# The first layer of a fused feed-forward, over pairs of token tiles with seven block products in place of eight

## The chip, the cores and the metric

The kernel runs on one core of a Trainium2 chip. The metric is the device time of one execution in microseconds (us); lower is better. TensorE (PE in the rows, PEld for its weight loads) does the matrix products, VectorE (DVE), ScalarE (ACT) and GpSimd (POOL) do elementwise work, and SyncE (SP) issues all DMAs.

## The reference

```python
# attention with decay: B, H, S, D = 4, 8, 768, 64
state = gamma * state + k_t (outer) v_t ;  y_t = scale * q_t @ state
x = y in the layout [3072 tokens, 512]
# first feed-forward, w_in [512, 1024], w_out [1024, 512]
h = x @ w_in
sm = softmax(h) ; solu = h * sm
ln = (solu - mean) / sqrt(var + 1e-6) * g_ln
y = ln @ w_out
# second feed-forward, w_in [512, 2048], w_out [2048, 512]
out = ((y @ w_in2) * cos(y @ w_in2)) @ w_out2
```

## The kernel before

There are two stages. Stage one takes the 3072 tokens in 24 tiles of 128 (4 sequences of 6 tiles) through attention and the first feed-forward, and stores y, transposed, to a scratch tensor. Stage two runs the second feed-forward over four blocks of 768 tokens; its first layer already uses a Strassen scheme. Every fp32 product is made of three matmuls of the fp32r kind: each operand is split in a high and a low part, and `products` (lines 318, 320, 321) issues high by high, high by low and low by high into one PSUM bank. ScalarE writes the high part with a copy, VectorE the low part with a subtraction.

The order of work in stage one is written by hand. A list STEP names the pieces of one step; all engines walk this same list, in order, each doing the pieces that it has, and a piece with number k works on tile n-k in step n. So each engine is a queue of its own, and they meet at semaphores only. The pieces that matter here, by engine:

- TensorE: L1a and L1b are the two halves (512 columns each) of h = x @ w_in, 12 matmuls each, into PSUM banks 4 and 5. T0 and T1 (L642) transpose the centred activations, four blocks each. OS, SC, DL, OP are the attention products. YT transposes y (L677). L2a and L2b are the second layer, 18 and 6 matmuls.
- VectorE: SM masks the scores, X makes the low part of x out of PSUM (L1084), L1b takes the row maximum of h out of PSUM (L1101), U multiplies h by its exponentials (L1107), CEN subtracts the mean (L1121), VAR (L1126, L1130) prepares the scale, T0 and T1 make the low part z_l (L1135), ST updates the state, YT copies y (L1147).
- ScalarE: X makes the high part of x, EX the exponentials, SQ the squares, T0 and T1 the high part of z, L2b the scaled copy of y out of PSUM (L808).
- GpSimd: PK and PV scale q and k (L973, L978), SG decays the state, VAR takes the power (L994).
- Preparing the weights of stage two rides along: in five of the six steps of a sequence (from step 4 on, 16 units in all) GpSimd forms four sums of 128x128 blocks (WS, L1018), ScalarE casts them (WH, L818 and L821), and VectorE makes the low parts: WD (L1150, 896 columns) at the end of a step, and WE (L1155, 512 columns) as its first piece in the next. In ScalarE's queue WH stands behind L2b.

Before step 4 each engine walks a list of its own (pe_first, act_first, dve_first, pool_first), in which the weights of the first feed-forward are loaded and split. `wait` and its relatives make an engine wait until a semaphore has counted to a tile's value.

## Time and profile before

| what | value |
|---|---|
| median of 3 runs | 895.1 us (894.12 to 895.19) |
| the profiled execution's own time | 894.13 us |
| its span, from first to last instruction | 892.3 us |
| granted TensorE clock, mean | 1.000 of full speed |
| TensorE busy | 884.3 us, 99% |
| VectorE busy | 588.7 us, 66% |
| ScalarE busy | 436.9 us, 49% |
| GpSimd busy | 148.0 us, 17% |

A matmul's shown duration contains the part in which it overlaps its neighbours in the pipeline, so it is longer than the distance from one start to the next, and a busy TensorE may still have short gaps. Times in the rows count from the span's start.

### The profile page before, as it was taken

The page shows a single profiled execution, that of the slowest core. Times are in us where ns is not written, and L with a number is a line of the kernel's source. Part 1 is how long each engine was busy: PE and PEld are TensorE (multiplying, and loading weights), DVE is VectorE, ACT ScalarE, POOL GpSimd, SP SyncE. Part 2 cuts the span into 40 slices and gives each one's busy share as a digit, 9 for nine tenths or more (in the row PEclk, how much of TensorE's full clock was granted, in tenths as well). Part 3 has the DMA queues.
Part 4 walks back from the last instruction along what each step waited for, and adds up shares of the span by engine and source line. Part 5 has one row for each costly group of instructions (what it writes and reads, how often), then busy time and mean ns, then how long its engine had stood idle before and what let it go on. Part 6 is the DMA issues. An engine that isn't in the chain of part 4 may idle for free.

```text
span 892.3 us, 14480 instructions
## 1 busy us (share of the span) xinstructions
PE 884.3 (99%) x5218; PEld 773.4 (87%) x5218; DVE 588.7 (66%) x849; ACT 436.9 (49%) x663; POOL 148.0 (17%) x186
## 2 busy tenths in 40 slices
PE   8999999999999999999999999999999999999998
PEld 6788888888888888889999999999999999999997
DVE  5865777577756777576666765566756658755654
ACT  2533433343334433465545755455655547564553
POOL 2332435234342442400000000000000000000000
PEclk9999999999999999999999999999999999999999
DMA  9534665456645563649854447344365434454301
GB/s 339 195 125 143 208 214 177 145 200 222 218 148 180 173 235 131 225 136 343 292 167 114 121 133 255 108 125 122 109 191 184 129 108 126 119 180 124 108 0 71
DMA packets 106662, 148.18 MB, mean 166 GB/s; under 512 B 7424, under 2 KB 77184, under 8 KB 106624
## 3 DMA queue, kind: packets, MB, share of 16 engines
q1 hardware_dynamic: 106624, 147.69, 51.6%
q8 instruction: 21, 0.34, 0.2%
q14 instruction: 17, 0.14, 0.1%
HBM read 112.01 MB, written 35.65 MB: 165 GB/s over the span
## 4 chain that ended last, share of the span: by engine, by line
PE 96%; DVE 1%; DMA 1%; SPq 1%; issue 0%; ACT 0%; POOL 0%; POOLq 0%; ACTq 0%
PE bank L318 28%; PE bank L321 28%; PE bank L320 28%; PE bank L557 3%; PE bank L642 2%; PE bank L606 2%; PE bank L589 2%; PE bank L677 2%; PE bank L577 1%; DMA w_raw<-w_in 1%; DVE w1i_l L1090 0%; DVE w1o_l L1095 0%; DMA out<-o_a 0%; SPq L419 0%; DVE nmax L1101 0%
## 5 line engine op out<-in xcount | busy, mean ns | idle before, releaser
L318 PE MATMUL bank<-yc_h,ring 128*128 128x384 f32 x448 | 151.5, 338 | 0.0
L320 PE MATMUL bank<-yc_l,ring 128*128 128x384 f32 x448 | 151.3, 338 | 0.0
L321 PE MATMUL bank<-yc_h,ring 128*128 128x384 f32 x448 | 150.9, 337 | 0.0
L1184 DVE SCALAR_TENSOR_TENSOR gg<-turns,c 128x768 f32<-128x768 int32 x64 | 61.0, 954 | 63.8 <-ACT turns L849 63.8
L855 ACT ACTIVATE gg<-gg 128x768 f32<-128x768 f32 x64 | 54.1, 846 | 80.2 <-DVE gg L1191 80.1
L849 ACT ACTIVATE turns<-c 128x768 int32<-128x768 f32 x64 | 54.2, 846 | 79.1 <-DVE c L1254 76.6
L318 PEld LDWEIGHTS bank<-yc_h,ring 128*128 128x128 f32 x448 | 84.2, 188 | 7.9 <-issue 0.5
L320 PEld LDWEIGHTS bank<-yc_l,ring 128*128 128x128 f32 x448 | 84.2, 188 | 7.2
L321 PEld LDWEIGHTS bank<-yc_h,ring 128*128 128x128 f32 x448 | 84.1, 188 | 0.0
L318 PE MATMUL bank<-w1i_h,x_h 128*128 128x512 f32 x192 | 77.8, 405 | 1.2 <-DVE w1i_l L1090 0.9
L318 PE MATMUL bank<-w1o_h,z_h 128*128 128x512 f32 x192 | 77.1, 401 | 0.0
L321 PE MATMUL bank<-w1i_h,x_l 128*128 128x512 f32 x192 | 75.2, 392 | 0.0
L321 PE MATMUL bank<-w1o_h,z_l 128*128 128x512 f32 x192 | 75.1, 391 | 0.0
L321 PE MATMUL bank<-w2o,glo_l 128*128 128x512 f32 x192 | 75.0, 391 | 0.0
L320 PE MATMUL bank<-w2o,glo_h 128*128 128x512 f32 x192 | 75.0, 391 | 0.0
L320 PE MATMUL bank<-w2o,ghi_h 128*128 128x512 f32 x192 | 74.9, 390 | 0.0
L320 PE MATMUL bank<-w1i_l,x_h 128*128 128x512 f32 x192 | 74.9, 390 | 0.0
L321 PE MATMUL bank<-w2o,ghi_l 128*128 128x512 f32 x192 | 74.8, 390 | 0.0
L320 PE MATMUL bank<-w1o_l,z_h 128*128 128x512 f32 x192 | 74.8, 389 | 0.0
L318 PE MATMUL bank<-w2o,glo_h 128*128 128x512 f32 x192 | 74.6, 389 | 0.0
L318 PE MATMUL bank<-w2o,ghi_h 128*128 128x512 f32 x192 | 74.6, 388 | 0.0
L803 ACT CAST z_h<-bank 128x512 fp32r<-128x512 f32 x48 | 28.2, 587 | 91.2 <-PE bank L642 91.1
(101 smaller groups left out, 1724.5 us busy)
## 6 DMA issues: line engine op xcount, KB each, us to landing
ring<-w_split SPq DMA_DIRECT2D x224, 256.0 KB, 2.8
w_split<-w_out SPq DMA_DIRECT2D x16, 896.0 KB, 4.2
w2o_split<-wo_out SPq DMA_DIRECT2D x16, 512.0 KB, 4.6
w2o<-w2o_split SPq DMA_DIRECT2D x8, 1024.0 KB, 8.4
raw<-qT SPq DMA_DIRECT2D x24, 256.0 KB, 3.0
raw<-kT SPq DMA_DIRECT2D x24, 256.0 KB, 2.7
raw<-kn SPq DMA_DIRECT2D x24, 256.0 KB, 3.7
raw<-vn SPq DMA_DIRECT2D x24, 256.0 KB, 4.8
```

What stands on the lines that cost most here:

```text
L318: eng.matmul(dst, ah, bh, start=first and i == 0, stop=False, skip_group_check=read_between)
L320: eng.matmul(dst, ah, bl, start=False, stop=False, skip_group_check=read_between)
L321: m = eng.matmul(dst, al, bh, start=False, stop=last_one and i == n - 1, skip_group_check=read_between)
L557: m = pe.matmul(ps_p[:, p, a, :], raw[rows(a), t % RAW, 1, cols], raw[rows(a), t % RAW, 0, cols], start=True, stop=True, tile_position=(a ...
L589: pe.matmul(ps_o[:, p, :], s_32[:, (t % TILES - 1) % 2, p, :, :].rearrange("p a n -> p (a n)"), raw[:, t % RAW, 0, p * C:(p + 1) * C], sta ...
L606: m = pe.matmul(ps_o[rows(a), p, :], raw[:, t % RAW, 3, h], p_m[:, p // 2, o], start=p == 0 and t % TILES == 0, stop=p == PAIRS - 1, tile_ ...
L642: m = pe.transpose(ps_t[:, k * 128:(k + 1) * 128], c_b[:, (4 * g + k) * 128:(4 * g + k + 1) * 128], ident[:, :])
L677: m = pe.transpose(ps_t[:, k * 128:(k + 1) * 128], y32[:, k * 128:(k + 1) * 128], ident[:, :])
L803: act.copy(z_h[:, 4 * g:4 * g + 4, :].rearrange("p k t -> p (k t)"), ps_t[:, :])\
L849: act.activation(turns[:, r, :], flat(c_32[:, r, :, :]), ACT.Copy, scale=INV_2PI)\
L855: act.activation(gg[:, r, :], gg[:, r, :], ACT.Sin, scale=0.5)\
L1184: dve.scalar_tensor_tensor(gg[:, r, :], turns[:, r, :], -TWO_PI_HI, flat(c_32[:, r, :, :]), ALU.mult, ALU.add)\
```

## The change

The first layer of the first feed-forward is computed for two token tiles at a time. x of a pair is cut in four blocks of 128 tokens by 256 features, w_in in four blocks of 256 by 512. Seven products P1, P2, P6, P5, P7, P3, P4 (the Winograd form of Strassen's scheme) take the place of eight; each is six matmuls of 512 columns. They alternate between bank_x and bank_y, and h is put together from them: ScalarE copies P1, P1+P6 and P5 out of PSUM (f_a, f_b) and the last sum as a quarter of h; VectorE adds three quarters (h11, h12, h22) into SBUF, where h now lies. The maximum, the exponentials and U read h from SBUF.

Four sums of x blocks are formed by GpSimd (XS), the high parts by ScalarE (in X and XH), the low parts by VectorE (XE, XL). The four sums of w_in blocks are formed by GpSimd at the start (TS), and the seven weight blocks are split in WVH and WVL in place of W1H and W1L; w_out of the first feed-forward is split in step 4 (WOH, WOL). In a step of odd n TensorE runs PA (P1, P2) and PB (P6, P5), in one of even n PC (P7) and PD (P3, P4). All pieces behind the first layer come two steps later. The tail, in which the first products of stage two fill in, is written for the six steps from 24 to 29. The SBUF plan is new; one quarter of w_out is loaded over a weight sum, so its load waits for the weight split.

The core of the diff (the lists before step 4 are of TensorE, ScalarE, VectorE and GpSimd, in this order):

```diff
-STEP = [("PK", 0), ("PV", 0), ("SG", 1), ("WE", 1), ("L1a", 2), ("T0", 3), ("L1b", 2),
-        ("T1", 3), ("EX", 2), ("OS", 1), ("SC", 0), ("DL", 1), ("OP", 1), ("YT", 4), ("U", 2), ("SM", 0), ("X", 1),
-        ("ST", 1), ("WS", 0), ("L2a", 3), ("SQ", 2), ("L2b", 3), ("CEN", 2),
-        ("VAR", 2), ("WH", 0), ("WD", 0)]
-LAG = 4
+STEP = [("PK", 0), ("PV", 0), ("SG", 1), ("WE", 1), ("MO", 4), ("PA", 3), ("PC", 4), ("T0", 5),
+        ("PB", 3), ("PD", 4), ("ME", 4), ("T1", 5), ("EX", 4), ("OS", 1), ("SC", 0), ("DL", 1),
+        ("OP", 1), ("YT", 6), ("U", 4), ("SM", 0), ("X", 1), ("XE", 1), ("ST", 1), ("XS", 1),
+        ("WS", 0), ("L2a", 5), ("SQ", 4), ("XH", 1), ("L2b", 5), ("CEN", 4), ("XL", 1), ("VAR", 4),
+        ("WH", 0), ("WD", 0)]
+LAG = 6
...
+                    ("OS", 1), ("OP", 1), ("DL", 1), ("PA", 0), ("SC", 2), ("OS", 2), ("DL", 2),
+                    ("OP", 2), ("PB", 0), ("SC", 3)]
+        act_first = [("WVH", 0), ("X", 0), ("WVH", 1), ("X", 1), ("PA", 0), ("WVH", 2), ("XH", 1),
+                     ("WVH", 3), ("WVH", 4), ("X", 2), ("PB", 0), ("WVH", 5), ("WVH", 6)]
+        dve_first = [("QS", 0), ("ID", 0), ("SC0", 0), ("SC1", 0), ("QS", 1), ("ST", 0),
+                     ("WVL", 0), ("XE", 0), ("SC0", 1), ("SC1", 1), ("ST", 1), ("WVL", 1),
+                     ("WVL", 2), ("PA", 0), ("SC0", 2), ("SC1", 2), ("XL", 1), ("WVL", 3),
+                     ("ST", 2), ("WVL", 4), ("XE", 2), ("WVL", 5), ("WVL", 6), ("SC0", 3),
+                     ("SC1", 3)]
+        pool_first = [("NS", 0), ("NS", 1), ("TS", 0), ("SG", 1), ("XS", 1), ("QS", 2), ("NS", 2),
+                      ("TS", 1), ("SG", 2), ("QS", 3), ("NS", 3)]
+        head, tail = [], []
...
+                    if u == KD:
+                        sp.wait_ge(w1i_lo, ORDER.index(P6) + 1)
+                        sp.wait_ge(ws_done, 4)
...
+                elif name == "PA" and par == 0:
+                    l1(b, t, P1)
+                    l1(b, t, P2)
+                elif name == "PB" and par == 0:
+                    l1(b, t, P6)
+                    l1(b, t, P5)
+                elif name == "PC" and par == 0:
+                    l1(b, t, P7)
+                elif name == "PD" and par == 0:
+                    l1(b, t, P3)
...
+                if p == P1:
+                    pair_wait(pe, xa_lo, b, m)
+                    pair_wait(pe, h21_done, b, m - 1)
+                elif p == P2:
+                    pair_wait(pe, h12_done, b, m - 1)
+                elif p == P6:
+                    pair_wait(pe, xs_lo, b, m)
+                    pair_wait(pe, f1_done, b, m)
+                elif p == P5:
+                    pair_wait(pe, h11_done, b, m)
+                elif p == P7:
+                    pair_wait(pe, f2_done, b, m)
+                elif p == P3:
+                    pair_wait(pe, f5_done, b, m)
+                else:
+                    pair_wait(pe, h22_done, b, m)
+                x, w = XPART[p], ORDER.index(p)
+                products(pe, bank_y if p in (P2, P5, P3) else bank_x, [
+                    (xv_h[:, x, k, :], xv_l[:, x, k, :], w1i_h[:, w, k, :], w1i_l[:, w, k, :])
+                    for k in range(2)], p in (P1, P2, P5), True, True).then_inc(l1_done, 1)
...
+                    pair_wait(act, xs_lo, b, m - 1)
+                    act.copy(xs[:, 2 * par:2 * par + 2, :, :].rearrange("p a k t -> p (a k) t"),
+                             ps_o).then_inc(x_done, 1)
+                    if par == 0:
+                        wait(act, x_done, b, t)
+                        l1_wait(act, b, m - 1, P2)
+                        act.copy(xv_h[:, 0:2, :, :], xs[:, XA11:XA12 + 1, :, :])\
+                            .then_inc(xa_hi, 1)
+                elif name == "XH" and par == 1:
+                    wait(act, x_done, b, t)
+                    pair_wait(act, xs_done, b, m, 4, 3)
+                    l1_wait(act, b, m - 1, P4)
+                    act.copy(xv_h[:, 2:7, :, :], xs[:, XA22:, :, :]).then_inc(xs_hi, 1)
+                elif name == "PA" and par == 0:
+                    l1_wait(act, b, m, P1)
+                    pair_wait(act, h22_done, b, m - 1)
+                    act.copy(f_a[:, :], bank_x).then_inc(f1_done, 1)
+                elif name == "PB" and par == 0:
+                    l1_wait(act, b, m, P6)
+                    pair_wait(act, h12_done, b, m - 1)
+                    act.copy(f_b[:, :], bank_x).then_inc(f2_done, 1)
+                    l1_wait(act, b, m, P5)
+                    pair_wait(act, h11_done, b, m)
+                    act.copy(f_a[:, :], bank_y).then_inc(f5_done, 1)
+                elif name == "PD" and par == 0:
+                    l1_wait(act, b, m, P4)
+                    wait(act, cen_done, b, t - 1)
+                    act.copy(h_of[1][:, 0:512], bank_x).then_inc(h21_done, 1)
...
+                elif name == "XS" and par == 1:
+                    m = t // 2
+                    wait(pool, x_done, b, t)
+                    pair_wait(pool, xs_lo, b, m - 1)
+                    combine(xs[:, XS1, :, :], xs[:, XA21, :, :], xs[:, XA22, :, :], ALU.add)\
+                        .then_inc(xs_done, 1)
...
+                elif name == "TS":
+                    if t == 0:
+                        pool.wait_ge(ld_w1[0], 16)
+                        pool.wait_ge(ld_w1[1], 16)
+                        combine(sum_1, q12, q11, ALU.subtract).then_inc(ws_done, 1)
+                        pool.wait_ge(ld_w1[2], 16)
+                        pool.wait_ge(ld_w1[3], 16)
+                        pool.wait_ge(ws_done, 1)
+                        combine(sum_2, q22, sum_1, ALU.subtract).then_inc(ws_done, 1)
+                    else:
+                        combine(q12, q22, q12, ALU.subtract).then_inc(ws_done, 1)
+                        pool.wait_ge(ws_done, 2)
+                        pool.wait_ge(w1i_lo, ORDER.index(P2) + 1)
+                        combine(q21, q21, sum_2, ALU.subtract).then_inc(ws_done, 1)
...
+                elif name == "XE" and par == 0:
+                    pair_wait(dve, xa_hi, b, m)
+                    dve.tensor_tensor(xv_l[:, 0:2, :, :], xs[:, XA11:XA12 + 1, :, :],
+                                      xv_h[:, 0:2, :, :].bitcast(F32), ALU.subtract)\
+                        .then_inc(xa_lo, 1)
+                elif name == "XL" and par == 1:
+                    pair_wait(dve, xs_hi, b, m)
+                    dve.tensor_tensor(xv_l[:, 2:7, :, :], xs[:, XA22:, :, :],
+                                      xv_h[:, 2:7, :, :].bitcast(F32), ALU.subtract)\
+                        .then_inc(xs_lo, 1)
+                elif name == "PA" and par == 0:
+                    l1_wait(dve, b, m, P2)
+                    pair_wait(dve, f1_done, b, m)
+                    wait(dve, sq1_done, b, t - 2)
+                    dve.tensor_tensor(h_of[0][:, 0:512], bank_y, f_a[:, :], ALU.add)\
+                        .then_inc(h11_done, 1)
+                elif name == "PC" and par == 0:
+                    l1_wait(dve, b, m, P7)
+                    pair_wait(dve, f5_done, b, m)
+                    wait(dve, sq1_done, b, t - 1)
+                    dve.tensor_tensor(h_of[1][:, 512:1024], bank_x, f_a[:, :], ALU.add)\
+                        .then_inc(h22_done, 1)
+                elif name == "PD" and par == 0:
+                    l1_wait(dve, b, m, P3)
+                    pair_wait(dve, f2_done, b, m)
+                    dve.tensor_tensor(h_of[0][:, 512:1024], bank_y, f_b[:, :], ALU.add)\
+                        .then_inc(h12_done, 1)
...
+                elif name in ("ME", "MO") and par == int(name == "MO"):
+                    if par:
+                        pair_wait(dve, h21_done, b, m)
+                        pair_wait(dve, h22_done, b, m)
                     else:
+                        pair_wait(dve, h11_done, b, m)
+                        pair_wait(dve, h12_done, b, m)
+                    dve.tensor_reduce(nmax[:, par:par + 1], h_of[par], AX.X, ALU.max,
                                       negate=True).then_inc(nm_done, 1)
                 elif name == "U":
                     wait(dve, e_done, b, t)
+                    dve.scalar_tensor_tensor(h_of[par], h_of[par], 1.0, e_b, ALU.mult, ALU.mult,
```

## Rows read from the trace of the kernel before

**Rows 1.** Busy time by window: from:to us, length, PE, PEld, DVE, ACT, POOL, clock
```profile
200.00:220.00 20.00, 20.00 (x137) 16.36 (x137) 15.65 (x23) 6.84 (x11) 10.75 (x12) 1.00 0.58 198
380.00:400.00 20.00, 20.00 (x111) 17.91 (x110) 14.29 (x25) 12.95 (x21) 0.74 (x2) 1.00 0.44 134
```

**Rows 2.** Costliest groups, the first layer's: count, busy us, mean ns of one
```profile
L318 PE MATMUL bank<-w1i_h,x_h 128*128 128x512 f32 x192 | 77.8, 405 | 1.2 <-DVE w1i_l L1090 0.9
```

**Rows 3.** Timeline of TensorE over one step: start us, us, engine, line, operation
```profile
197.55 0.39 PE L318 MATMUL bank<-w1i_h,x_h 128*128 128x512 f32 x1
...
200.28 0.60 PE L642 MATMUL bank<-ident,work 128*128 128x128 f32 x4
...
203.58 0.66 PE L642 MATMUL bank<-ident,work 128*128 128x128 f32 x4
...
207.64 0.66 PE L677 MATMUL bank<-ident,work 128*128 128x128 f32 x4
208.05 0.47 PE L318 MATMUL bank<-w1o_h,z_h 128*128 128x512 f32 x1
...
213.62 0.39 PE L318 MATMUL bank<-w1i_h,x_h 128*128 128x512 f32 x1
```

**Rows 4.** Timeline of ScalarE at the same step's start
```profile
197.75 0.69 ACT L808 ACTIVATE work<-bank,scl 128x512 f32<-128x512 f32 x1 [2.10 <-PE bank L321]
198.34 0.93 ACT L818 CAST w_out<-w_raw 128x896 fp32r<-128x896 f32 x1
199.17 0.62 ACT L821 CAST wo_out<-wo_raw 128x512 fp32r<-128x512 f32 x1
```

**Rows 5.** Timeline of VectorE in the same step
```profile
198.10 0.15 DVE L1130 TENSOR_SCALAR scl<-scl 128x1 f32<-128x1 f32 x1
199.30 2.05 DVE L1150 TENSOR_TENSOR w_out<-w_raw,w_out 128x896 fp32r<-128x896 f32 x1 [1.05 <-ACT w_out L818]
201.27 1.53 DVE L1155 TENSOR_TENSOR wo_out<-wo_raw,wo_out 128x512 fp32r<-128x512 f32 x1
202.83 0.69 DVE L1135 TENSOR_TENSOR z_l<-bank,z_h 128x512 fp32r<-128x512 f32 x1
203.69 1.23 DVE L1101 TENSOR_REDUCE nmax<-bank 128x1 f32<-128x1024 f32 x1 [0.16 <-PE bank L321]
```

**Rows 6.** Timeline of GpSimd in the same step
```profile
198.33 0.55 POOL L994 TENSOR_TENSOR scl<-scl,mhalf 128x1 f32<-128x1 f32 x1 [5.97 <-DVE scl L1130]
...
199.10 1.30 POOL L973 TENSOR_TENSOR raw<-raw,cst 128x512 f32<-128x512 f32 x1
200.35 1.90 POOL L978 TENSOR_TENSOR raw<-raw,cst 128x512 f32<-128x512 f32 x1
```

**Rows 7.** All instructions of four lines: duration ns min/median/max, first and last start
```profile
L1150 DVE TENSOR_TENSOR w_out<-w_raw,w_out x16: 1175/2032/2067, 58.3 to 342.2; 128x896 fp32r<-128x896 f32 x16
L1155 DVE TENSOR_TENSOR wo_out<-wo_raw,wo_out x16: 1526/1528/1528, 60.0 to 344.1; 128x512 fp32r<-128x512 f32 x16
L978 POOL TENSOR_TENSOR raw<-raw,cst x24: 1038/1892/1902, 9.0 to 343.1; 128x512 f32<-128x512 f32 x24
L1018 POOL TENSOR_TENSOR w_raw<-w_raw x64: 452/457/465, 46.3 to 334.5; 128x128 f32<-128x128 f32 x64
L1018 POOL TENSOR_TENSOR y_raw<-y_raw,t x4: 1854/1856/1859, 374.3 to 745.7; 128x768 f32<-128x768 f32 x4
```

**Rows 8.** Timeline of the start: tile 3's inputs, w_in's split, tile 3's scores, step 5
```profile
15.77 0.40 SPq L415 DMA_DIRECT2D raw<-kT  x1
...
17.07 1.05 ACT L784 CAST w1i_h<-w_raw 128x1024 fp32r<-128x1024 f32 x1 [0.23 <-DMA w_raw<-w_in]
...
39.34 1.16 PE L557 MATMUL bank<-raw 64*128 64x128 f32 x16 [0.84 <-POOL raw L973]
...
56.50 0.39 PE L318 MATMUL bank<-w1i_h,x_h 128*128 128x512 f32 x1
```

**Rows 9.** DMA issues of the page: KB each, median us from issue to landing
```profile
raw<-kT SPq DMA_DIRECT2D x24, 256.0 KB, 2.7
```

More of the change, by code:

```diff
@@ L60 @@
 W1_UNITS = KD + K1 // 2
-W1_SLOTS = W1_UNITS
 RAW = 3
@@ L105, in build @@
         ps_d = bank[:, 3, 0:PAIRS * D].rearrange("p (c n) -> p c n", c=PAIRS)
-        ps_h = bank[:, 4:6, :]
+        bank_x, bank_y = bank[:, 4, :], bank[:, 5, :]
         ps_t = bank[:, 6, :]
@@ L233, in build @@
         o_stored = sem("o_stored")
-        late = {"T1": [("TA", 0)],
-                "CEN": [("YH", P1), ("YH", P2), ("YL", P1), ("YL", P2)]}
         def unit(b, n):
@@ L263, in build @@
-        for n in range(4, TILES):
-            head += [(name, n - behind) for name, behind in STEP]
-        body = [(name, n - behind) for n in range(TILES) for name, behind in STEP]
-        for name, behind in STEP:
-            if behind and name not in ("WE", "WS", "WH", "WD"):
-                tail.append((name, NT - behind))
-                tail += late.get(name, [])
-        last = NT - 1
-        tail += [("L1a", last), ("T0", last - 1), ("YH", P6), ("YL", P6), ("YH", P5), ("L1b", last),
-                 ("T1", last - 1), ("EX", last), ("P", P1), ("TBL", 0), ("LA", last - 1),
-                 ("U", last), ("CEN", last), ("P", P2), ("SQ", last), ("LB", last - 1),
-                 ("T0", last), ("YL", P5), ("VAR", last), ("YH", P3), ("P", P6), ("LC", last - 1),
-                 ("YH", P7), ("YT", last - 2), ("YL", P3), ("P", P5), ("YL", P7), ("LD", last - 1),
-                 ("T1", last), ("P", P3), ("LA", last), ("YH", P4), ("YL", P4), ("P", P7),
-                 ("LB", last), ("P", P4), ("YT", last - 1), ("LC", last), ("LD", last),
-                 ("Q", P1), ("YT", last), ("Q", P2)]
+                    ("OS", 1), ("OP", 1), ("DL", 1), ("PA", 0), ("SC", 2), ("OS", 2), ("DL", 2),
@@ new lines, in build @@
+        head, tail = [], []
+        outputs = {"U": 0, "ST": 1, "CEN": 2, "VAR": 3}
+        for n in range(4, TILES):
+            for name, behind in STEP:
+                if n >= behind:
+                    head.append((name, n - behind))
+                if n == 4 and name in outputs:
+                    head += [("WOH", outputs[name]), ("WOL", outputs[name])]
+        body = [(name, n - behind) for n in range(TILES) for name, behind in STEP]
+        late = {(25, "YT"): [("TA", 0)],
+                (26, "EX"): [("YH", P1), ("YL", P1)], (26, "U"): [("YH", P2), ("YL", P2)],
+                (26, "CEN"): [("YH", P6), ("YL", P6)],
+                (27, "T0"): [("YH", P5), ("TBL", 0), ("P", P1), ("YL", P5), ("P", P2)],
+                (27, "T1"): [("YH", P3), ("YL", P3)],
+                (27, "YT"): [("P", P6)],
+                (27, "L2b"): [("YH", P7), ("YL", P7)],
+                (28, "T0"): [("P", P5), ("YH", P4), ("YL", P4), ("P", P3)],
+                (28, "YT"): [("P", P7)],
+                (28, "L2b"): [("P", P4), ("Q", P1)]}
@@ L280, in wait @@
+        for n in range(NT, NT + LAG):
+            for name, behind in STEP:
+                if n - behind < NT and name not in ("WE", "WS", "WH", "WD"):
+                    tail.append((name, n - behind))
+                tail += late.get((n, name), [])
+        tail += [("Q", P2)]
         def wait(eng, s, batch, tile, per=1, i=0, per_batch=TILES):
@@ L293, in wait_state, with pair_wait, l1_wait @@
                  per_batch=TILES - 1)
+        def pair_wait(eng, s, batch, pair, per=1, i=0):
+            wait(eng, s, batch, pair, per, i, per_batch=PAIRS_IN)
+        def l1_wait(eng, batch, pair, p):
+            pair_wait(eng, l1_done, batch, pair, 7, ORDER.index(p))
         def wait_decay(eng, s, batch, tile):
@@ L469, in tile @@
                     load_next(t, (n + 2) % RAW)
-                store_yt(t - LAG)
-            sp.wait_ge(w1_lo, W1_UNITS)
-            for n in range(LAG, TILES):
+                if not isinstance(t, int) or t >= LAG:
+                    store_yt(t - LAG)
+            sp.wait_ge(w1i_lo, 7)
+            for n in range(4, TILES):
                 tile(0, n)
@@ L629, in step @@
                     if g == 0:
-                        if isinstance(b, int) and t == NT - 1:
-                            wait(pe, zl_done, b, t - 1, 2, 1)
-                        else:
-                            wait(pe, ytc_done, b, t - 2)
+                        wait(pe, ytc_done, b, t - 1)
+                        wait(pe, zl_done, b, t - 1, 2, 1)
                         if filling(t, b):
@@ L638, in step @@
                         wait(pe, zl_done, b, t, 2, 0)
-                        if isinstance(b, int) and t == NT - 1:
-                            wait(pe, ytc_done, b, NT - 3)
                     for k in range(4):
@@ L969, in step @@
                     wait(pool, q_sc, b, t - 1)
-                    if filling(t, b) and t > 1:
-                        pool.wait_ge(w1_lo, KD if t == 2 else W1_UNITS)
                     pool.tensor_tensor(q, q, qsc, ALU.mult).then_inc(q_sc, 1)
```

211 lines of the change are left out of this document (104 added, 107 removed), and 8 rows, old and new, of tables (dve_first, pe_first).

## The prediction

> **What bounds the kernel now.** The windows come first [rows 1]: in stage one TensorE is busy 20.00 of 20 us, VectorE 15.65, GpSimd 10.75, at a granted clock of 1.00. The bound is the issue of TensorE's queue. The groups of instructions [rows 2] say what the first layer costs, and here is a trap: 405 ns is the mean time of one, but they overlap. The timeline gives the price [rows 3]: 12 of them lie between 197.55 and 200.28, 2.73 us, so 0.2275 us each. The same timeline gives one step: 197.55 to 213.62, 16.07 us. What I time everything against is "+x", the time since TensorE's first matmul of a step.
>
> Then the other engines at a step's start. ScalarE copies y when the second layer has ended (+0.20) and only then casts the stage-two weights for WD (+0.79 to +1.72) and for WE (to +2.24) [rows 4]. VectorE has been done with VAR since +0.70, waits for that cast, runs WD from +1.75 to +3.80, WE to +5.25, and only then z_l at +5.28 [rows 5]. T1 on TensorE, the first thing that waits for z_l, starts at +6.03 [rows 3]. So before the change WD and WE end just in time; nothing that TensorE needs sooner stands behind them.
>
> Why they last so long: WE has 512 columns and takes 1.53 us in all 16 cases; WD takes 1.18 at least and 2.03 in the median [rows 7]. GpSimd's PK runs 199.10 to 200.40, its PV 200.35 to 202.25 [rows 6]. WD therefore works 0.95 us, after PK has ended, and WE 0.55 us, after PV; PV takes 1.89 in the median and 1.04 at least [rows 7]. They take turns.
>
> **The change, part by part.**
>
> *Removed on TensorE.* 48 matmuls for two tiles become 42: 72 fewer over 12 pairs, by 0.2275: 16.4 us. This is all that can be won. The seven products have the shapes of the old ones, so I give them the same price.
>
> *A new wait in even steps.* P4 accumulates onto bank_x and must wait for h22, which VectorE reads out of the same bank. Without waits TensorE comes to P4 after P7 (1.37), T0 (0.35) and P3 (1.37): +3.1. On VectorE h22 is queued behind WD and WE of the step before. These keep their place: the cast still stands behind L2b's copy, and VectorE's pieces before it sum to the same (XE of 512 columns for X), so PK comes when it came. WE ends at +5.25, h22 takes 0.6 (the distance at which z_l of 512 columns, shown as 0.69, lets its follower start), and P4 starts at about +5.9: 2.8 us lost. T0's and T1's z_l and ME stand behind h22, but P4 and its product last until +7.3, so they add nothing. Below: were the port free, WE would end at 1.75+0.95+0.55=3.25 and P4 would be 0.8 late. Above: 3.0. I take 2.8, by the row. The weight units exist in five steps of six; their WD stands ahead of an even step 6 times (steps 8, 10, 14, 16, 20, 22). 16.8 us.
>
> *A new wait in odd steps.* P5 starts bank_y anew and must wait for h11. TensorE would come to it after P1, P2, T0 and P6, at +4.5. VectorE has WD, WE, then MO (a maximum over 1024 columns, 1.15 us of distance [rows 5]), then h11 (0.6). But the step before held XL, 1280 columns, 1.36 us by WD's rate, in place of X's 0.68, behind a chain (x copy, four sums, cast): VAR ends at about +1.8 instead of +0.70. So WD starts at +1.8 with GpSimd not yet in PK and ends at +2.75. If WE comes after GpSimd's VAR and PK (0.77 and 1.25), it ends at 5.35, MO at 6.5, h11 at 7.1: 2.6 lost. If it slips in behind the first of them, at 3.85, MO ends at 5.0 and h11 at 5.6: 1.2 lost. I take 2.0, as I can't tell who wins. Below: port free throughout, 3.25+1.15+0.6=5.0, 0.6 lost. Above, 4.4, is the second rival. These are 10 steps (5, 7, 9 and so on to 23): 20 us. In odd steps f1, ScalarE's copy of P1, is ready at +2.8, before P6 at +3.1: nothing.
>
> *x sums.* XS is four sums of 256 columns. The rows have 128 columns in 0.457 and 768 in 1.856 us, so 2.18 ns a column: 0.74 each, 2.9 together [rows 7]. From the end of OP: x copy 0.6, sums 2.9, cast 1.3, XL 1.4: 6.2 us at least. P6 comes after YT and the second layer (0.4 and 5.6 us, from 207.64, 208.05 to 213.62 [rows 3]), P1, P2 and T0 (3.1): 9.1. Hidden by 2.9 us, 1.8 when U (1.14) holds the port; above, it is the second rival again. The other added copies (f1, f2, f5, h21, 0.6 each) and the maximum from SBUF lie on engines with room: VectorE's load for two tiles rises from some 25 us of 32 to some 27 of 36.
>
> *The start.* Before step 5 the new order has done 78 matmuls (17.7 us) and five groups of four transposes (2.0) less than the old one, which reached step 5 at 56.50 [rows 8]. It breaks even if it gets there at 36.8. But GpSimd now carries the weight sums: the last w_in rows are there at 17.07 [rows 8], a sum of 1024 columns is 2.4 us, so: second sum to 19.5, SG, XS, QS and NS of tiles 1 and 2 (about 6.2) to 25.7, two sums to 30.5. SyncE's load of a quarter of w_out waits for the last of them, and the inputs of tile 3, issued at 15.77 before [rows 8], stand behind it: issued at about 31, landed 2.7 us later [rows 9] and more with the quarter ahead, scaled by GpSimd in 1.3: SC of tile 3 at 36 to 37. From there to step 5 the old kernel took 17.2 us [rows 8]; the new one has 30 matmuls and three groups of transposes less, 8.0: step 5 at about 45.3, 8.5 lost. In step 5 P6 is due 3.1 us in and XL of tile 3, with the w_out splits between, ends some 6.5 us in: 3.5 more. Together 12; below 3 (only that last wait), above 17 (all four w_out splits, 1.37 each, ahead of XL).
>
> *The tail.* The work moved there meets a TensorE that is full [rows 1], with the products of stage two as filling as before. 1 us, from 0 to 4 (one elementwise chain not covered). Stage two is untouched.
>
> *The sum.* -16.4 + 16.8 + 20 + 12 + 1 = +33.4 us on the span of 892.3: 925.7. The execution took 894.13, 1.8 above its span, and the median is 895.1, 1.0 above that: 928. The bounds of the terms give 893.5 and 966.
>
> **The rivals.**
>
> *The waits are covered (faster).* P4 and P5 find h22 and h11 done. It decides at +3.1 and +4.5: if VectorE has h22 and h11 before. For it: VectorE idles 1.05 us ahead of WD [rows 5], and ScalarE is half idle. Against: the cast ends at +1.75 whatever VectorE does, and WD and WE need 1.5 behind it even alone. Then 892.3-16.4+4 (start)=880, 883 with the 2.8.
>
> *GpSimd's chain gets long.* WS now stands behind XS, and WH behind WS. Four x sums (2.9), four weight sums (1.8), and in between, one after the other, what VectorE does with the same port: U (1.14), CEN (0.7), XL (1.36). Begun 0.3 us after L2a's start, this ends at 8.3, 2.7 us into the odd step, where the cast began at +0.79: WD 1.9 later, and an odd step loses 4.4. That is 24 more: 952. For it: PV's 1.89 for 1.04 [rows 7]. Against: an engine waits at most one instruction of the other. The Trainium skill says as much (SBUF — State Buffer, Who interferes with whom): a VectorE instruction with two SBUF inputs and a GpSimd one that reads SBUF exclude each other for the whole instruction. By that rule U belongs to these only after the change, since its h came from PSUM before; the trace agrees for WD and WE, and no row shows it for U.
>
> *The waits are short.* GpSimd is out of the way in nearly all steps: 6 by 0.8, 10 by 0.6, start 12, tail 1: +7.4, 902.5. Against: the rows of WE, 1.53 in all 16.
>
> A fall of the granted clock in the new gaps has no row: it was 1.00 also at the start.
>
> **How the numbers follow.** Forecast 0.5, long chain 0.13, short waits 0.2, covered 0.12, something else 0.05 (spread over both sides). A measurement of this kernel can tell 0.2%, 1.8 us, from no change. Slower: 0.5+0.13+0.2 and part of the rest, 0.84. Faster 0.13, same 0.03. Range 892 to 950: from the lower sum of the terms to just below the long chain; it leaves out the covered case and part of the long chain.
>
> **What would show it.** Even steps: TensorE idle some 2.8 us ahead of a six-matmul group, released by VectorE's addition, and no such idle time in steps 12 and 18, whose step before has no weight unit. Odd steps: the same ahead of the fourth product. VectorE: WD, WE, then (MO and) an addition, back to back. Start: SC of tile 3 near 36, held by GpSimd, step 5 near 45. A pair of steps takes about 35.5 us, not 32.1. I am wrong if the pair takes 31 us, or if the addition ends before TensorE gets to its product; the sum is wrong in the start if step 5 begins by 38.

## The result and the profile after

The changed kernel took 998.2 us in the median of 4 runs (994.3 to 1010.4), the kernel before 894.9: ratio 1.114, interval 1.108 to 1.120 (1010.4 is an execution in a slower state, and the ratio leaves it out). It is slower by 103 us, and the range of the prediction ended at 950. The profiled execution of the changed kernel is that longest one, so the ledger below sums to 116 us of span, not to 103. The four spans go with the mean granted clock: 992.5 and 992.9 us at 0.971, 999.9 at 0.959, and the profiled 1008.6 at 0.951. The ledger therefore has a second measured column, from the run e4_sp_order below (996.85 us, clock 0.969), which differs from the changed kernel in the place of one load at the start and in nothing else.

The page first: busy time and share of the span, then the granted clock in 40 slices, and the first layer's group.

```profile
PE 911.9 (90%) x5146; PEld 789.9 (78%) x5146; DVE 639.5 (63%) x888; ACT 488.4 (48%) x740; POOL 222.4 (22%) x238
...
PE   6569878888888878898789999999999999999998
...
PEclk8879888999889998999699999999999999999999
...
L361 PE MATMUL bank<-w1i_h,xv_h 128*128 128x512 f32 x168 | 76.3, 454 | 59.6 <-DVE work L1209 27.0
```

Three things are to be seen. The group has 168 instructions for 192 [rows 2], so the 24 (and as many on each of the two other lines) are gone. Its idle time has grown from 1.2 us to 59.6. And the row of the clock, in slices of 25 us, has sevens and eights among its nines in the first 400 us, where the change is, and a six at 479 to 504, in the tail; behind that it has nines only. Before, it was 1.00 in the windows of stage one [rows 1].

TensorE's waits between 60 and 450 us: what waited, for whom, us in total, times, the longest.

```profile
PE bank L361 <- DVE work L1209: 27.0, 10, 3.0
PE bank L361 <- DVE work L1215: 16.1, 6, 2.7
PE bank L361 <- ACT f_a L851: 12.9, 10, 3.6
```

L1209 is h11, L1215 is h22, L851 is f1. The two waits of the prediction are there, 10 and 6 times as it counted them; the third is one that it had put at nothing.

**An even step.** TensorE begins it at 236.77; start, duration, line, and in brackets the idle time ahead and its releaser.

```profile
236.77 0.39 PE L361 MATMUL bank<-w1i_h,xv_h 128*128 128x512 f32 x1
...
242.80 0.50 PE L361 MATMUL bank<-w1i_h,xv_h 128*128 128x512 f32 x1 [2.67 <-DVE work L1215]
243.14 0.39 PE L363 MATMUL bank<-w1i_l,xv_h 128*128 128x512 f32 x1
243.37 0.39 PE L364 MATMUL bank<-w1i_h,xv_l 128*128 128x512 f32 x1
```

VectorE in the same stretch:

```profile
238.52 2.05 DVE L1290 TENSOR_TENSOR w_out<-w_raw,w_out 128x896 fp32r<-128x896 f32 x1 [1.04 <-ACT w_out L902]
240.50 1.53 DVE L1295 TENSOR_TENSOR wo_out<-wo_raw,wo_out 128x512 fp32r<-128x512 f32 x1
242.06 0.69 DVE L1215 TENSOR_TENSOR work<-bank,f_a 128x512 f32<-128x512 f32 x1
```

WD at +1.75, WE at +3.73, h22 at +5.29, P4 at +6.03: these are the times of before [rows 5], and h22 stands behind them as forecast.

**An odd step.** It begins at 254.28. TensorE:

```profile
254.28 0.39 PE L361 MATMUL bank<-w1i_h,xv_h 128*128 128x512 f32 x1
...
258.55 0.47 PE L361 MATMUL bank<-w1i_h,xv_h 128*128 128x512 f32 x1 [0.94 <-ACT f_a L851]
...
262.92 0.80 PE L361 MATMUL bank<-w1i_h,xv_h 128*128 128x512 f32 x1 [2.75 <-DVE work L1209]
263.51 0.63 PE L363 MATMUL bank<-w1i_l,xv_h 128*128 128x512 f32 x1
263.94 0.63 PE L364 MATMUL bank<-w1i_h,xv_l 128*128 128x512 f32 x1
...
265.65 1.05 PE L680 MATMUL bank<-ident,work 128*128 128x128 f32 x4
```

What the other engines did ahead of it: GpSimd, ScalarE, VectorE.

```profile
249.08 3.94 POOL L1130 TENSOR_TENSOR xs<-xs 128x256 f32<-128x256 f32 x4 [6.16 <-ACT xs L836]
252.99 3.44 POOL L1130 TENSOR_TENSOR w_raw<-w_raw 128x128 f32<-128x128 f32 x4
```
```profile
256.46 0.94 ACT L902 CAST w_out<-w_raw 128x896 fp32r<-128x896 f32 x1 [1.28 <-POOL w_raw L1130]
...
257.82 0.58 ACT L851 COPY f_a<-bank 128x512 f32<-128x512 f32 x1
```
```profile
257.43 2.13 DVE L1290 TENSOR_TENSOR w_out<-w_raw,w_out 128x896 fp32r<-128x896 f32 x1 [0.95 <-ACT w_out L902]
259.49 1.53 DVE L1295 TENSOR_TENSOR wo_out<-wo_raw,wo_out 128x512 fp32r<-128x512 f32 x1
260.94 1.21 DVE L1242 TENSOR_REDUCE nmax<-work 128x1 f32<-128x1024 f32 x1
262.18 0.69 DVE L1209 TENSOR_TENSOR work<-bank,f_a 128x512 f32<-128x512 f32 x1
```

Read it from the end. P5 waits for h11, h11 for WD, WE and the maximum, WD for the cast of w_out (+2.18 here, +0.79 in the even step), the cast for the four weight sums, and those begin only when the four x sums are over. The same cast stands ahead of f1 on ScalarE, so P6 waits too. And after the gap the matmuls of P5 come to follow each other by 0.43 us, where P6 ahead of the gap and P4 behind the even step's gap kept 0.23. The windows say why: length, busy times of PE, PEld, DVE, ACT, POOL, and the third number from the end is the granted clock.

```profile
240.00:245.00 5.00, 2.33 (x14) 1.89 (x14) 4.87 (x6) 0.50 (x2) 2.92 (x2) 1.00 0.68 231
260.00:265.00 5.00, 2.25 (x6) 1.69 (x6) 3.43 (x4) 0.59 (x1) 2.28 (x3) 0.71 0.90 320
265.00:270.00 5.00, 5.00 (x40) 4.36 (x41) 0.69 (x1) 2.31 (x4) 1.37 (x4) 0.61 0.19 74
```

The clock fell from 2.4 to 1.2 GHz in this gap, and stayed there for some us in which TensorE was busy all the time.

**The ledger.** "Work" is the changed kernel's without a wait: the steps of before less 0.2275 us for each matmul removed. TensorE's first matmul of step 6 and of step 24 cut the span in three.

| us | predicted | measured | in e4_sp_order |
|---|---|---|---|
| matmuls removed | -16.4 | -16.4 | -16.4 |
| start, to step 6 (work 52.2, took 86.4) | +14 | +34.2 | +33.8 |
| even steps' wait, 6 | +16.8 | +17.4 | +17.4 |
| odd steps' waits, 9 (7 to 23) | +18 | +37.1 | +37.1 |
| clock in steps 6 to 24 | 0 | +20.2 | +10.0 |
| tail, step 24 to the end (work 552.0, took 576.3) | +1 | +24.3 | +20.8 |
| sum | +33 | +117 | +103 |

The predicted 20 for ten odd steps is put here as 18 and, for step 5, 2 in the start. The waits and the clock are kept apart by the run e6_busy_both below. So most of what the profiled execution has more than e4's is clock: 10 us of it in the steps.

### The profile page after: what moved, and what is told of

Read it like the earlier page. It is cut to its first block, busy times and chain, and to the rows that moved or that the text cites. A ratio compares the mean times of both kernels' runs of the same rounds, so it can differ in the third digit from the quotient of the medians.

```text
span 1008.6 us, 14770 instructions
## 1 busy us (share of the span) xinstructions
PE 911.9 (90%) x5146; PEld 789.9 (78%) x5146; DVE 639.5 (63%) x888; ACT 488.4 (48%) x740; POOL 222.4 (22%) x238
## 4 chain that ended last, share of the span: by engine, by line
PE 69%; issue 13%; POOL 8%; DVE 5%; ACT 3%; DMA 1%; SPq 1%; POOLq 0%; ACTq 0%; DVEq 0%
PE bank L361 21%; PE bank L363 20%; PE bank L364 20%; POOL w_raw L1130 4%; PE bank L604 2%; PE bank L636 2%; PE bank L653 2%; DVE wo_out L1295 2%; POOL xs L1130 1%; PE bank L680 1%; DVE nmax L1242 1%; POOL raw L1059 1%; PE bank L703 1%; PE bank L624 1%; DMA w_raw<-w_in 1%
## 5 line engine op out<-in xcount | busy, mean ns | idle before, releaser
L361 PE MATMUL bank<-yc_h,ring 128*128 128x384 f32 x448 | 153.4, 342 | 3.9 <-ACT c L1019 2.3
L364 PE MATMUL bank<-yc_h,ring 128*128 128x384 f32 x448 | 152.4, 340 | 0.0
L361 PE MATMUL bank<-w1i_h,xv_h 128*128 128x512 f32 x168 | 76.3, 454 | 59.6 <-DVE work L1209 27.0
L361 PEld LDWEIGHTS bank<-yc_h,ring 128*128 128x128 f32 x448 | 85.2, 190 | 12.5 <-issue 5.3
L361 PEld LDWEIGHTS bank<-w1i_h,xv_h 128*128 128x128 f32 x168 | 34.6, 206 | 76.2 <-DVE work L1209 31.6
L1130 POOL TENSOR_TENSOR y_raw<-y_raw,t 128x768 f32<-128x768 f32 x4 | 7.9, 1967 | 377.7 <-DVE yc_l L1306 377.7
L364 PEld LDWEIGHTS bank<-yc_h,ring 128*128 128x128 f32 x448 | 85.3, 190 | 0.0
L364 PE MATMUL bank<-w2o,ghi_l 128*128 128x512 f32 x192 | 74.8, 390 | 0.0
L364 PE MATMUL bank<-w1i_h,xv_l 128*128 128x512 f32 x168 | 72.1, 429 | 0.0
```

The lines of the kernel that those rows point to most:

```text
L361: eng.matmul(dst, ah, bh, start=first and i == 0, stop=False, skip_group_check=read_between)
L364: m = eng.matmul(dst, al, bh, start=False, stop=last_one and i == n - 1, skip_group_check=read_between)
L1130: return pool.tensor_tensor(dst, a, b, op)
```

## The experiments

In order of the steps they test. Each time is a median of four and stands beside 894.8 for the kernel before. "Start", "steps" and "tail" are the three parts of the ledger in the profiled execution.

| kernel | us | start | steps 6 to 24 | tail |
|---|---|---|---|---|
| before | 894.9 | 72.4 | 284.0 | 535.9 |
| changed | 998.2 | 86.4 | 345.9 | 576.3 |
| work alone | | 52.2 | 271.7 | 552.0 |
| e1_we_later | 941.0 | 81.2 | 282.7 | 576.3 |
| e2_ws_first | 965.1 | 85.5 | 307.0 | 570.5 |
| e3_busy | 1011.4 | 86.8 | 348.3 | 575.0 |
| e4_sp_order | 995.6 | 86.0 | 336.2 | 572.8 |
| e6_busy_both | 1000.0 | 86.5 | 332.6 | 575.0 |
| e7_both | 967.2 | 79.5 | 309.4 | 576.2 |
| e8_tail | 959.3 | 80.1 | 310.0 | 567.6 |
| e9_start | 966.0 | 78.5 | 309.6 | 576.3 |
| e10_wh_later | 930.3 | 82.4 | 271.1 | 576.2 |
| e11_tail1 | 927.3 | 81.4 | 282.5 | 560.7 |
| e12_best | 912.8 | 76.0 | 271.1 | 560.7 |

**Do WD and WE hold h22 and h11 up?** In STEP both go behind T1:

```
-STEP = [... ("SG", 1), ("WE", 1), ("MO", 4), ... ("T1", 5), ("EX", 4), ... ("WH", 0), ("WD", 0)]
+STEP = [... ("SG", 1), ("MO", 4), ... ("T1", 5), ("WD", 1), ("WE", 1), ("EX", 4), ... ("WH", 0)]
```

> On VectorE the two weight pieces WD and WE move from the seam of two steps to behind T1's z_l of the next step, where VectorE idles for some 2.8 us; nothing else moves. Theory A (what stands in front of h22 and h11 in VectorE's queue sets the waits): in even steps h22 is ready before P4 is due, so the 2.8 us ahead of P4 vanish (6 times); in odd steps only MO and h11 remain, but P6 still waits for f1, which stands on ScalarE behind the late cast: some 1.5 us lost in place of 4; the clock stays at 1.00 in stage one. Together 60 to 75 us less than the changed kernel's 998: 923 to 938, with the start's loss left in. Theory B (VectorE's load and the turns it takes with GpSimd set the waits, whatever the order): within 10 us of 998.

940.97 us, ratio 1.050 (1.045 to 1.054): 57 won by moving two instructions, a little under the 60 to 75 expected. VectorE in this kernel, h22 and then WD and WE:

```profile
239.57 0.69 DVE L1215 TENSOR_TENSOR work<-bank,f_a 128x512 f32<-128x512 f32 x1 [0.69 <-PE bank L364]
...
244.50 1.08 DVE L1290 TENSOR_TENSOR w_out<-w_raw,w_out 128x896 fp32r<-128x896 f32 x1
245.50 0.69 DVE L1295 TENSOR_TENSOR wo_out<-wo_raw,wo_out 128x512 fp32r<-128x512 f32 x1
```

h22 no longer waits for anything but TensorE. WD takes 1.08 for 2.05 and WE 0.69 for 1.53: away from GpSimd's PK and PV they need half the time. The one wait left in the steps is f1's, 1.15 us in the mean of eight odd steps:

```profile
PE bank L361 <- ACT f_a L851: 9.2, 8, 1.5
```

**Does the chain over the sums make the odd step late?** The weight sums go ahead of the x sums:

```
-        ("OP", 1), ... ("XE", 1), ("ST", 1), ("XS", 1), ("WS", 0), ("L2a", 5), ...
+        ("OP", 1), ... ("XE", 1), ("ST", 1), ("WS", 0), ("XS", 1), ("L2a", 5), ...
```

> On GpSimd the weight sums WS go ahead of the x sums XS; nothing else moves. If the long chain (XS, then WS, then the cast, then WD) causes the longer loss of odd steps: the cast starts at +0.8 again, the wait for f1 ahead of P6 vanishes, h11 comes 2 us earlier, 10 times, and most clock falls go too: 20 us alone, up to 50 with the clock: 948 to 978. The even steps' 2.8 us stay. If the chain is not the cause (only WD and WE themselves): within 5 us of 998.

965.06, ratio 1.078 (1.075 to 1.080). The odd steps took 16.2 and 17.0 us for 19.2 to 22.9, and h11's wait fell to 0.8; h22's stayed at 2.7. The time lies within the 948 to 978 expected.

```profile
PE bank L360 <- DVE work L1214: 13.4, 5, 2.7
PE bank L360 <- DVE work L1208: 6.5, 8, 0.9
```

So the odd steps' excess over the forecast is the order of the sums on GpSimd: the rival "GpSimd's chain gets long" had happened. With this order an odd step lost 0.9 to 1.1 us, less than the 2.0 of the forecast. The even steps with a weight unit all took 18.9 to 19.1 us here, some 1.5 more than the 17.5 that their work and their wait make at the full clock (e6_busy_both below).

**What does the clock cost?** First with 20 small fp32 matmuls between P6 and P5, to keep TensorE busy in the gap.

```
                     l1(b, t, P6)
+                    keep_busy(20)
                     l1(b, t, P5)
```

> 20 small matmuls (128 columns, into the idle PSUM bank of y, on a constant) between P6 and P5, about 2.9 us by the rate of the warm-up matmuls at the start (8 in 1.16 us): they fill the gap ahead of P5 and leave its cause alone. Clock theory (TensorE's idle time in odd steps is what lowers the granted clock, and half speed after it costs about 3 us each time): the granted clock is near 1.00 from step 6 to 24, the gaps stay as long, and the time falls by 20 to 30 us: 968 to 978. Rival (the clock falls for another reason, or the low clock costs nothing as the engine waits anyway): within 5 us of 998, or slower by up to 6 where the small matmuls delay P5.

1011.38, ratio 1.129: no gain, a miss. The fillers took 4.6 us, not 2.9, so they outlasted the gap. The odd steps then ran at the full clock, but in the even ones it now fell in all six (it had fallen in four), here in the step that answers to the one shown above, behind the same gap of 2.67:

```profile
243.88 0.80 PE L361 MATMUL bank<-w1i_h,xv_h 128*128 128x512 f32 x1 [2.67 <-DVE work L1222]
```

The length of one gap does not decide it, then. The second try put 10 in both gaps, some 2.3 us, which is less than the gap:

```
+                    keep_busy(10, ps_y[:, 0:128])
                     l1(b, t, P5)
...
+                        keep_busy(10, bank[:, 0, 0:128])
                     l1(b, t, P4)
```

> The changed kernel with ten small matmuls (about 2.3 us by the run before, where 40 instructions took 4.62) in both gaps, ahead of P5 and ahead of P4, so shorter than the gaps (2.75 and 2.67 us) and cut of no wait. In steps without a gap they cost 2.3 us each (about 8 of them, 18 us). Clock theory: the clock stays at 1.00 between steps 6 and 24, which gives back 20 to 28 us; together 988 to 1000, with a mean clock above 0.985. Rival (the falls come whatever stands in the gaps): the mean clock stays at 0.97 and the time rises to about 1015.

999.99, ratio 1.118 (1.116 to 1.120), the changed kernel's time within the intervals, and at the end of the 988 to 1000 expected. But now, in its profiled execution, each odd step took 19.2 or 20.1 us and each even one with a weight unit 17.5, without exception, and the clock was 1.00 in both windows, 100 to 240 and 240 to 400, of which the first is shown (the three even steps without a weight unit took 16.3 for 14.1, since there the fillers meet no gap):

```profile
100.00:240.00 140.00, 132.76 (x956) 112.58 (x956) 98.53 (x150) 60.48 (x97) 68.69 (x80) 1.00 0.48 162
```

In the changed kernel the same steps took 19.2 to 22.9 and 17.5 to 20.4. This run gives the price of the waits alone: 17.5 less 14.6 of work is 2.9, 19.2 less 15.0 and 20.1 less 16.0 is 4.1. The changed kernel's steps with a gap either took exactly these times or 1.2 to 2.9 us more: more in 10 of 15, 20.2 in all (12.8 in odd, 7.4 in even steps). In e4_sp_order, where the same steps have the same waits, it is 6 of 15 and 10.0 us. So 20 us is what the clock took in the longest execution, and 10 in one near the median. That is why the medians are alike: the fillers give these 10 back, but cost 6.7 us in the three steps without a gap and some 2 in the tail (575.0 for 572.8). The profiled execution of e6 (995.85) is also the fastest of its four and alone above the mean clock of 0.985 that was expected; the three others, 999.9 to 1000.5, had 0.978. That the clock stayed up in their steps as well is not shown.

**The two edits together**, WD and WE later and the weight sums first:

> WD and WE behind T1's z_l, and WS ahead of XS, together. Theory: what was left in odd steps of the first of the two edits alone, the wait for f1 behind the late cast (about 1.5 us, 10 times), goes: 925 to 930, and a pair of steps takes 30.8 us, the sum of TensorE's work, so that the seven products are worth their 16 us between steps 6 and 24. Rival: another wait (h11, or x's low parts ahead of P6) takes its place and the time stays at 938 to 941.

967.21, ratio 1.081: 26 us worse than the first edit alone, and a plain miss. Three of the nine odd steps took 15.0 us, but the other six took 21.4 to 23.4. GpSimd in that kernel:

```profile
262.15 2.17 POOL L1129 TENSOR_TENSOR w_raw<-w_raw 128x128 f32<-128x128 f32 x4 [7.55 <-DMA w_raw<-w_in]
264.28 2.94 POOL L1129 TENSOR_TENSOR xs<-xs 128x256 f32<-128x256 f32 x4
```

WD later frees the raw weights later, so the next block is loaded later, and the weight sums, which now stand first, hold the x sums behind a DMA. On ScalarE f1 stands behind the cast of these sums, and P6 waits for f1; XL, which P6 needs too, had ended about 1 us before the wait did:

```profile
271.07 0.76 PE L360 MATMUL bank<-w1i_h,xv_h 128*128 128x512 f32 x1 [3.63 <-ACT f_a L850]
```

The x sums took 2.94 here, with VectorE idle beside them, and 3.94 in the changed kernel. That the two edits work against each other was not in the expectation; each was right for the order that it was made in.

**f1.** So the weight sums stay behind, and instead the cast WH moves off f1's way, on top of the first edit:

```
-        ("PB", 3), ("PD", 4), ("ME", 4), ... ("VAR", 4), ("WH", 0)]
+        ("PB", 3), ("PD", 4), ("WH", 1), ("ME", 4), ... ("VAR", 4)]
```

> Edit: WD and WE behind T1 as in the run that had them there alone (940.97 us), and ScalarE's cast WH moved from the end of the step to behind PD of the next, so that it no longer stands in front of f1. That run's odd steps took 16.4 and 17.5 us, 1.4 above their work (15.0 and 16.07), and the only wait of TensorE in them was 1.0 to 1.2 for f1. Theory: f1 stands behind WH, and WH waits for GpSimd's weight sums. With WH behind it the nine odd steps from 7 to 23 lose their 1.4: 12.6 us, and steps 6 to 24 take 270 to 273: 926 to 930. Rival: TensorE's product P6 needs XL too, which runs behind the four x sums and its own cast; with f1 gone it waits for XL instead, and the gain is under 4 us: 937 to 941.

930.30, ratio 1.039 (1.036 to 1.041). It is what was expected (926 to 930), and P6's need of XL, the rival, brought no wait. Steps 6 to 24 took 271.1 us, their work (271.7, before's own small waits included). The odd steps are 15.3 and 15.9, the even 14.1 and 14.6, a pair up to 30.5, and nothing of the three waits is left:

```profile
240.00:340.00 100.00, 99.78 (x724) 83.93 (x718) 76.33 (x137) 53.06 (x84) 54.62 (x68) 1.00 0.58 199
```

This settles the middle: three pieces of weight preparation (WD, WE, WH) in the wrong place cost the 74.8 us that the changed kernel's steps took above these, the clock's 20 included.

**The start.** SyncE's load of the last quarter of w_out goes behind the inputs of tiles 3 and 4:

```
-            load_w1(KD)
             load_next(1, 0)
             load_next(2, 1)
+            load_w1(KD)
```

> In SyncE's queue the load of the last quarter of w_out goes behind the inputs of tiles 3 and 4. My step of the start: the inputs of tile 3 come in 8 to 10 us earlier, so SC of tile 3 starts some 8 us earlier than at 45.6, and step 5 begins at about 48 to 50: 6 to 9 us less, 989 to 992. Rival: the start is held by GpSimd's sums and the split of the weights anyway, and at most 3 us are won.

995.57, ratio 1.111. The inputs of tile 3 were issued at 24.91 for 37.89, and its scores began at 40.99 for 45.60, but step 6 came 0.4 us earlier and no more. Between them TensorE now waits for others:

```profile
40.99 1.16 PE L604 MATMUL bank<-raw 64*128 64x128 f32 x16 [0.48 <-POOL raw L1054]
45.74 0.50 PE L361 MATMUL bank<-w1i_h,xv_h 128*128 128x512 f32 x1 [2.00 <-DVE w1i_l L1224]
```

The rival held. Then the lists of the start were reordered as well, on top of the two edits together (ScalarE's x copy ahead of the first cast, VectorE's scores ahead of the first difference, two splits of w_out earlier):

```
-        act_first = [("WVH", 0), ("X", 0), ("WVH", 1), ("X", 1), ...
+        act_first = [("X", 0), ("WVH", 0), ("X", 1), ("WVH", 1), ...
```

> The same as the run with both edits, and the lists before step 4 in another order: ScalarE takes x of tile 0 and 1 ahead of the weights' high parts, VectorE the masks of tile 1 ahead of the weights' low parts, GpSimd q and k of tile 2 ahead of XS, SyncE tile 3's and 4's inputs ahead of the last quarter of w_out, and two of the four w_out splits come before step 4. Theory: the start loses its 34 us to single waits in those orders (4.6, 2.2, 5.5, 3.3, 3.6 and 3.0 us of TensorE's idle time) and to half speed after them: 12 to 20 us less, 907 to 915. Rival: the work on GpSimd and VectorE itself (sums, 11 units of 1024 columns to split) bounds the start: under 6 us less.

966.02 against 967.21: again a miss. The first 20 us went better (TensorE busy 14.45 us for the changed kernel's 12.48), then the waits came back one by one, and the windows show who is full:

```profile
20.00:40.00 20.00, 12.02 (x90) 8.92 (x90) 15.64 (x12) 10.27 (x15) 19.92 (x14) 0.83 0.65 233
40.00:60.00 20.00, 16.53 (x89) 12.44 (x90) 16.41 (x23) 5.63 (x10) 7.88 (x10) 0.66 0.21 70
```

GpSimd is busy 19.92 of the 20 us up to 40, and VectorE some 16 in each window. From this I read that the weight sums and splits bound a large part of the start, whatever their order; no run took them away, so it is not shown. On top of e10's steps the same lists were worth more, 5.4 to 6.3 us of start in the last run below, with a clock of 0.91 for 0.66 in 40 to 60.

**The tail.** YT goes behind L2a in the steps past the last tile:

```
+        order = [x for x in STEP if x[0] != "YT"]
+        order.insert([x[0] for x in order].index("L2a") + 1, ("YT", 6))
         for n in range(NT, NT + LAG):
-            for name, behind in STEP:
+            for name, behind in order:
```

> The same as the run with both edits, and in the tail alone (steps 24 to 29) YT moves behind L2a on all engines. Theory: in the tail no attention work lies between T1 and YT, so YT waits for z_l of T1 (1.4 us shown, four times) and the clock falls after it; with the 12 matmuls of L2a between, these waits go: 8 to 14 us less than without, 913 to 920. Rival: the tail's loss is ScalarE's and VectorE's load, and at most 3 us go.

959.32 against 967.21: 7.9 won, just short of the 8 to 14 expected (the absolute figures had been worked out from a base that turned out 40 too low). YT's waits of 1.40 and 1.45 for z_l are gone. Left was CEN, behind the stage-two splits of P6 and P7. So these moved too, on top of the first edit:

```
-                (26, "CEN"): [("YH", P6), ("YL", P6)],
+                (26, "VAR"): [("YH", P6), ("YL", P6)],
...
-                (27, "L2b"): [("YH", P7), ("YL", P7)],
+                (27, "VAR"): [("YH", P7), ("YL", P7)],
```

> Edit: WD and WE behind T1 (940.97 us alone), and in the tail steps only YT behind L2a instead of behind OP, and the stage-two splits YH/YL of P6 and P7 moved behind VAR, so that z_l, CEN and VAR do not wait behind them. The run without this edit took 576.3 us from step 24 to the end, where the work is 552.0; it showed 11 us of waits for z_l and for CEN between 388 and 455, and a granted clock of 0.83 and 0.66 in 400 to 440. Theory: the tail's loss is these waits and the clock that falls behind them; 14 to 22 us are won: 919 to 927. Rival: the stage-two splits are late instead (the first product of stage two waits for them), and the gain is at most 8 us, as in the run that moved YT alone: 933 or more.

927.30, ratio 1.037 (1.035 to 1.038): 13.7 won where 14 to 22 were expected, and the tail is 560.7 for 576.3, 15.6 less.

**All of it:**

> Edit: WD, WE and WH later, the tail edit (YT, YH, YL), and the reordered first lists of the start. If the terms add: 940.97 less 12.6 (f1), less 14 to 22 (tail), less 1 (start, as the other run of it showed): 905 to 913. Of its 17 us or so above the ideal of 878.5 (894.9 less 16.4) nearly all would then be the start. Rival: a faster order gives up in one place what it wins in another, as when WS came first with WD and WE later; then 920 or more. In no case is it under the kernel before, 894.9.

912.77 us, ratio 1.020 (1.019 to 1.022), at the top of the 905 to 913 expected. (The expectation's "17 us or so" above the ideal was a slip: 905 to 913 lie 26 to 34 above its 878.5.) The first layer's group and the clock in this kernel:

```profile
PEclk9799999999999999999999999999999999999999
...
L363 PE MATMUL bank<-w1i_h,xv_h 128*128 128x512 f32 x168 | 70.8, 421 | 18.9 <-DVE w1i_l L1226 8.1
```

The idle time of the group is 18.9 for 59.6, and it lies in the start: between 100 and 340 us TensorE waits 0.5 us in all. Above the work stand 23.8 us of start and 8.7 of tail; the 16.4 won do not pay for them. The kernel before stays the fastest of all.

## Why the prediction was wrong

The sign was right, the size was not: 928 forecast, 998 measured. By the ledger's column of e4_sp_order 69 us are missing, in four terms: the start 19.8, the tail 19.8, the odd steps 19.1, and the clock, which had no term, 10.0 (20.2 in the longest execution). The bounds were added up wrongly as well: the lowest terms give 892.5, not 893.5, and the highest 961.7, not 966. Either way 998 lies above the highest of them.

*Removed on TensorE: right.* 72 matmuls, 0.2275 each; e10's steps took their work so computed.

*Even steps: right, in mechanism and size.* 2.8 forecast, 2.9 measured in e6, h22 behind WD and WE at the forecast times, and e1 removed it by moving these.

*Odd steps: the mechanism right, the size too small.* 2.0 forecast, 4.1 measured; WD began at +3.15, where the forecast had +1.8. Here the prediction had the right answer in its hands as the second rival, at 4.4 us an odd step, and gave it 0.13. The argument against it was that an engine waits for at most one instruction of the other. That may hold each time, but the sums are eight instructions: four x sums took 3.94 where 2.9 was forecast, four weight sums 3.44 for 1.8, and so the cast was 1.4 us late. And the term left out that ScalarE does that cast ahead of f1: "nothing" was 0.94 for P6, which is part of the 4.1. The rule of the Trainium skill cited there (SBUF — State Buffer, Who interferes with whom) was the better guide: it says that the lock holds for a whole instruction, and it does not say that a chain meets it once. The x sums took 2.94 with VectorE idle and 3.94 beside U (1.22 us), which of VectorE's larger pieces there is the only one with both inputs in SBUF; WD took 2.05 beside PK and 1.08 apart from it. That agrees with exclusion for U too, though no run has U alone beside the sums.

*The clock: put at nothing, without a reason that holds.* The prediction dismissed it in one sentence, "it was 1.00 also at the start". But in the whole trace of before, TensorE's longest wait between two of its instructions is 0.95 us, so that trace could not show what a gap of 2.7 does. It should have been an unknown with two ends, 0 and the doubled distance of the matmuls behind each gap. It took 20.2 us in steps 6 to 24 of the profiled execution and 10.0 in e4's, and a part of the start (clock 0.84, 0.83, 0.66 in the windows from 20 to 80) and of the tail (0.84 in 450 to 500), which was not separated. The Trainium skill warns of this (TensorE: Matmul & The Clock Gate, A second HAM failure mode: psum-queue depth-cycling): a kernel whose TensorE idles briefly and often between groups of matmuls can swing between the two clocks, and loses throughput in between. It says so of a bf16 kernel and gives no price. The trace agrees, with 0.71 and 0.61 behind the gap at 260, and the prediction should have had it as a rival.

*The start: too small, 14 for 34.2.* The chain that ended last ahead of tile 3's scores was the one described: tile 3's inputs behind SyncE's load of the last quarter of w_out.

```profile
12.09 25.70 SPq L438 DMA_DIRECT2D work<-w_out x2
37.89 0.41 SPq L458 DMA_DIRECT2D raw<-kT  x1
```

It released them at 37.9 instead of 31, and tile 3's scores came at 45.60, not 36.5. That is 9 of the 20. But e4 shows that this chain was only the last of several of nearly one length: its scores came 4.6 us earlier and step 6 only 0.4. GpSimd and VectorE carry the weight sums and splits, and without the one wait others take its place. The other 11 lie behind it, most in step 5, which took 29.7 us for the 15.9 of its work: three waits for CEN, f1 and h11, 9.9 us, and a clock of 0.66. The prediction summed durations on one engine as though the other were idle. How the 34 us divide between the load of these engines, the orders and the clock stays open; of all orders tried, the last run's was the best, with 23.8.

*The tail: 1 for 24.3.* "A TensorE that is full" was the wrong picture; in the last steps no new tile's work lies between the products, and the elementwise chains lie open. "One elementwise chain not covered" were six waits, 11 us together, three more ahead of products of stage two, 3.9 us, and for the rest the clock behind them (before, TensorE waits for nothing in this stretch); two of the six:

```profile
453.26 0.66 PE L703 MATMUL bank<-ident,work 128*128 128x128 f32 x4 [1.45 <-DVE z_l L1275]
...
491.54 1.09 PE L680 MATMUL bank<-ident,work 128*128 128x128 f32 x4 [3.25 <-DVE work L1261]
```

e11's order alone takes 15.6 of the 24.3 back.

## What to carry to other kernels

An instruction that ended just in time is a debt: when a change puts a new reader behind it, count every engine's queue from the first sum to the last, and where the only argument against a long chain is that exclusion costs "one instruction at most", count it once for each instruction of the chain. Where TensorE had no idle time before, a trace of before can't price a gap: beside the gap itself give the slower clock behind it a term of its own, from 0 up to as much again as the work that follows takes; here it was 0 or 1.2 to 2.9 us a gap. And what is moved to a start or a tail must be walked through with the queues of that start or tail, since there no steady work covers it.

## What the runs showed of the hardware

- Gaps of some 2.7 us cost more than themselves, in some steps and not in others of the same kernel: behind the one at 240 us the matmuls followed at 0.23 us, behind that at 260 at 0.43, and a step took 1.2 to 2.9 us more. This befell 10 of 15 such steps in one execution and 6 of 15 in another of the same order. Small matmuls in the gaps kept the clock at 1.00 between 100 and 400 us (the profiled execution of e6_busy_both). What decides in a given gap stays open: in e3_busy it fell in all six even steps, whose gap was the same as before, and in no odd one.
- Without such gaps the clock stays: 1.00 in all of steps 6 to 24 in e10_wh_later.
- Small fp32 matmuls of 128x128 took 0.23 us each (20 in 4.6), as long as one of the first layer's with 512 columns.
- ScalarE loaded its table just ahead of its first instruction, and only when that one's input had come: 1.28 us at 14.39. Where x, in place of the weights, stood first (e12_best), the same load ran at 0.96 us, and the x copy came at 10.05 for 16.64:

```profile
14.39 1.28 ACT L870 ACT_TABLE_LOAD   x1 [14.39 <-DMA w_raw<-w_in]
15.68 1.04 ACT L870 CAST w1i_h<-w_raw 128x1024 fp32r<-128x1024 f32 x1
```
